# Half of the hidden product moved between the score products of a solu/MoE kernel

## What is computed

```python
# attention: B, H, S, D = 4, 8, 768, 48
for t in range(S):
    S_re, S_im = ar * S_re - ai * S_im + kv[t], ar * S_im + ai * S_re
    y[t] = q[t] @ S_re
# dense layer: 3072 tokens, d_model 384, d_ff 1024
h = x @ w_in
e = exp(h - max(h));  solu = h * e / sum(e)
ln = (solu - mean) / sqrt(var + 1e-6) * g_ln
x = ln @ w_out
# experts: 8, hidden 1024, each token goes to its best two
out[token] += weight * (relu(x @ w1[e]) @ w2[e])
```

## Time and profile before

| | |
|---|---|
| median of 3 runs | 1293.69 us (1292.68 to 1297.07) |
| profiled execution, whole time | 1297.07 us |
| its span | 1295.3 us |
| TensorE busy | 1098.5 us (85%) |
| VectorE busy | 871.4 us (67%) |
| ScalarE busy | 621.1 us (48%) |
| mean granted TensorE clock | 0.942 of full |

### The profile page before, as it was taken

How to read it: one execution, slowest core, us unless ns; L and a number is a source line. 1 busy time by engine, 2 the same in 40 slices (tenths; PEclk the granted TensorE clock), 3 DMA queues, 4 the chain that set the end, 5 groups by cost and what they waited for, 6 DMA issues and landing times.

```text
span 1295.3 us, 21866 instructions
## 1 busy us (share of the span) xinstructions
PE 1098.5 (85%) x7864; PEld 982.9 (76%) x7864; DVE 871.4 (67%) x1715; ACT 621.1 (48%) x964; POOL 446.2 (34%) x416
## 2 busy tenths in 40 slices
PE   0016889988988988999995299999999999999996
PEld 0015667766766767777884299999999999999996
DVE  4849649948957966974542467777767776767772
ACT  4331454455445455353432255555555555555551
POOL 3020131224234233423342424444344444444431
PEclk9976979989989998999997599999999999999998
DMA  9320031130112021011110667677767776766740
GB/s 254 122 73 19 19 92 40 36 92 26 50 41 77 25 62 32 26 48 46 50 20 13 221 203 250 230 232 248 244 225 250 251 230 239 237 228 221 242 159 1
DMA packets 85979, 167.50 MB, mean 129 GB/s; under 512 B 18566, under 2 KB 57696, under 8 KB 85872
## 3 DMA queue, kind: packets, MB, share of 16 engines
q1 hardware_dynamic: 72432, 137.71, 33.5%
q0 software_dynamic: 13440, 28.40, 6.2%
HBM read 148.83 MB, written 21.92 MB: 132 GB/s over the span
## 4 chain that ended last, share of the span: by engine, by line
PE 52%; DVE 3%; issue 1%; ACT 1%; DMA 1%; POOL 1%; SPq 0%; POOLq 0%; DVEq 0%; ACTq 0%
PE bank L1301 21%; PE bank L1482 20%; PE bank L1358 3%; PE bank L1327 3%; PE bank L1292 2%; PE bank L1349 1%; PE bank L1397 1%; PE bank L1399 1%; PE bank L1426 0%; DVE turn L941 0%; DMA mine<-tags 0%; POOL tags L568 0%; DMA xg<-xs,mine 0%; DVE zl L1104 0%; PE bank L1379 0%
## 5 line engine op out<-in xcount | busy, mean ns | idle before, releaser
L854 ACT ACTIVATE hh<-bank 128x256 fp32r<-128x256 f32 x248 | 95.3, 384 | 253.9 <-PE bank L1301 253.9
L1301 PE MATMUL bank<-sxh,w1h 128*128 128x256 f32 x744 | 212.2, 285 | 1.9 <-DVE sxl L1247 1.9
L1301 PE MATMUL bank<-sxh,w1l 128*128 128x256 f32 x744 | 210.5, 283 | 0.0
L1301 PE MATMUL bank<-sxl,w1h 128*128 128x256 f32 x744 | 210.2, 282 | 0.0
L1270 DVE SCALAR_TENSOR_TENSOR hl<-bank,hh 128x256 fp32r<-128x256 f32 x248 | 104.8, 423 | 117.4 <-ACT hh L854 117.4
L646 POOL DMA_INDIRECT out<-yo,mine x62 | 77.9, 1257 | 275.9 <-DVE yo L1263 266.5
L1482 PE MATMUL bank<-w2h,hh 128*128 128x384 f32 x496 | 167.5, 338 | 0.0
L1482 PE MATMUL bank<-w2l,hh 128*128 128x384 f32 x496 | 166.7, 336 | 0.0
L1482 PE MATMUL bank<-w2h,hl 128*128 128x384 f32 x496 | 166.5, 336 | 0.0
L1301 PEld LDWEIGHTS bank<-sxh,w1h 128*128 128x128 f32 x744 | 140.6, 189 | 2.3 <-DVE sxl L1247 2.3
L1301 PEld LDWEIGHTS bank<-sxh,w1l 128*128 128x128 f32 x744 | 141.7, 190 | 0.0
(11 more groups left out here) (183 smaller groups left out, 2427.2 us busy)
## 6 DMA issues: line engine op xcount, KB each, us to landing
raw<-in_w SPq DMA_DIRECT2D x62, 1536.0 KB, 7.0
ar<-in_a_re SPq DMA_DIRECT2D x6, 768.0 KB, 4.5
turn<-in_a_im SPq DMA_DIRECT2D x6, 768.0 KB, 5.8
qk<-in_q SPq DMA_DIRECT2D x48, 96.0 KB, 2.4
qk<-in_k SPq DMA_DIRECT2D x48, 96.0 KB, 2.5
out<-wide SPq DMA_DIRECT2D x9, 512.0 KB, 11.4
vt<-in_v SPq DMA_DIRECT2D x24, 192.0 KB, 2.7
xs<-x SPq DMA_DIRECT2D x24, 192.0 KB, 2.7
```

Source lines behind the costliest of these rows:

```text
L854: nc.scalar.activation(hh[:, f % NH, :], bank[:, f % 2, 0:CAP], ACT.Relu).then_inc(hh_done, 1)
L1301: ins = MM(dst, stationary[a_](cc), moving[b_](cc), start=(n_ == 0), stop=(n_ == len(terms) - 1))
```

## The change

The hidden products are issued in two parts. The first half (12 products, bank 4) stays in front of the waits for the scores. The second half (12 products, bank 5) goes behind those waits, in three groups of four between the four pairs of score products; where there is no tile m, all of it follows directly. The group after p_ = 2 holds the last hidden product, which raises h_mm, so h_mm comes before the last quarter of the scores. a_mm is raised by the last score, as before.

```diff
-                    hidden(0, 6 * NP)
+                    hidden(0, 3 * NP)
                 if has(m):
 
                     pe.wait_ge(qp_done, 2 * (m + 1))
@@
-                    ins.then_inc(a_mm, 1)
+                        if p_ == NP - 1:
+                            ins.then_inc(a_mm, 1)
+                        else:
+                            hidden(3 * NP + NP * p_, 3 * NP + NP * (p_ + 1))
+                else:
+                    hidden(3 * NP, 6 * NP)
```

## The result

The changed kernel takes 1364.81 us (median of 4 runs, 1352.96 to 1370.98) against 1293.18 us beside it: 71.6 us slower by these medians. The ratio 1.0512 (95% interval 1.0428 to 1.0599), some 66 us, is that of the fast runs: it leaves out one execution in the slower state, 1370.98 us, and takes in three more, the profiled one among them. The forecast was slower, 1330 us, with a range of 1312 to 1348. The direction holds; the size is about twice the forecast. The profiled execution took 1354.94 us (span 1353.2), one of the quicker ones.

A forecast was written before the change was run, and what follows sets the result against it. TensorE's program order was taken to set the pace of most first-phase tiles, VectorE's queue in some. Terms 13.8 + 9.4 + 16.2 - 4 = +35.4 us, 36 added to the median 1293.69: about 1330 us, range 1312 to 1348.

The forecast's parts named there:

- The wait for zl moves: TensorE waits behind 12 hidden products instead of 24; where zl is late, 2.76 us more idle: 13.8 + 9.4 us.
- bodies of the first kind: Bodies 4, 8, 12, 16, 20, where zl is late; delay paid in full, 5 x 2.76 = 13.8 us.
- the second kind: Bodies 5, 9, 13, 17, zl late by less; some 0.4 us of slack before xl, so 9.4 us.
- Passages: Three added round trips a tile between hidden products and scores, 0.3 us each: 18 x 0.9 = 16.2 us.
- the last bodies: Bodies 21 to 24, nothing prepared for a later chunk, no wait for zl; expected to grow about 0.9 us each.
- The rival of free passages: Switching between scores and hidden products costs nothing: 1313 us, chance 0.12.
- h_mm later: The nmax reduction on VectorE starts later, covered by ScalarE's at; costed at nothing.
- TensorE's clock: Low clock after late zl stays as before; body 4's long low stretch becomes less likely: credit of 4 us.
- the clock turns against it: Longer pauses keep TensorE low through scores, half the hidden products and into the result part: 1353 us, chance 0.10.
- Absorbed: VectorE and ScalarE take up the delay in bodies 5, 9, 13, 17: 1320 us, chance 0.08.
- faster: Scores run under neighbouring hidden products in 18 tiles: 1284 us, chance 0.04.
- no change: Same overlap at about 1.2 us a tile, or gain and loss of like size; chance 0.04.

The follow-up runs named there:

- the single trip alone: Changed kernel with the second half of the hidden products as one block between score pairs 0,1 and 2,3: 1327.68 us, +37.9 against the kernel before.
- scores in one block: Kernel before with 12 hidden products ahead of the waits, then all scores unbroken, then the other 12 hidden products: 1326.84 us, +37.0.
- The two partial kernels: The new order only in the nine bodies where zl is late (1340.54 us, +49.5), or only in the other bodies (1315.27 us, +24.3).
- wait only: Kernel before with the waits moved behind 12 hidden products, the other 12 next, then the scores unbroken: 1317.33 us, +27.5.
- thin groups: Kernel before with 21 hidden products ahead of the waits and a single one in each of three gaps between score pairs: 1375.74 us, +85.9.
- the state block: State products issued together ahead of the result products: kernel before 1283.38 us, with zl early 1274.44, thin groups 1323.21, changed kernel 1338.11.

## Why the prediction was wrong in size

- **The wait for zl moves.** Right in place and size of the wait: 54.4 us in nine times, forecast 54. The price was forecast at 13.8 + 9.4 = 23.2 us; moved alone it costs 27.5. In that kernel the bodies of the first kind (but for body 4, whose long low stretch did not come) grew from xl to xl by some 3.5 instead of 2.76 us and the second kind by 2.9 to 3.7 instead of 2.4, because the 12 hidden products behind the pause run at 1.2 GHz: 5.05 us in body 12 instead of 2.76, 2.3 us lost, where the scores lost 1.7 before.
- **Passages.** 0.3 us a trip, measured 0.37 in the last bodies; 0.9 us a tile against 1.15. The bounds of 0.2 and 0.41 a trip hold there; the single trip alone cost 0.52, above them. That bodies 6, 10, 14 and 18 are covered by VectorE's queue was wrong: they pay 0.95 us through the slower pieces beside GpSimd. 18 x 1.15 + 4 x 0.95 = 24.5 us instead of 16.2. The rule of the Trainium skill ("TensorEngine Tiling (Array Packing)", Key Properties: a change of tiling mode drains TensorE) agrees with this: the 0.37 us stand in the trace, and the order that adds no change between 64 and 112 rows (scores in one block) left the period at 17.68 us. The rival of free passages has fallen.
- **h_mm later.** The wait before nmax is there in 20 bodies, and in the last bodies it costs nothing, as said: they grow by the trips alone.
- **TensorE's clock. This is the step that failed.** The prediction read from body 9 that the low stretch ends some 3.4 us after work resumes, left it at that for the new order, expected long stretches to become less likely because a block twice as long stands behind the wait, and credited 4 us. In the alternated block the clock stayed low for 4.1 to 10.2 us. In the two profiles that costs 29.8 - 12.4 = 17.4 us, near the 15 us that the prediction gave as the other end (low for twice as long); the absence of body 4's long stretch gives 5 of it back, for which the prediction had reckoned 6.7. So a loss of 12.4 us stands where a gain of 4 was entered. On the medians, 71.6 - 27.5 - 24.5 = 19.6 us is left for the clock (14 by the ratio), worked out and not measured by itself. The two partial kernels place it: in the nine late bodies 49.5 - 27.5 - 9 x 1.15 = 11.7 us, in the others 24.3 - 9 x 1.15 - 4 x 0.95 = 10.1 (differences of medians, so good to a few us). The rival "the clock turns against it" had 0.10 and 1353 and came nearest. Its size was about right; its cause was not, since it put the low clock down to the longer pauses, and these alone left it low for no more than 5.1 us.
- **Absorbed, faster, no change:** fell. Nothing was absorbed in bodies 5, 9, 13 and 17, which grew by 4.6 to 6.4 us from xl to xl.
- **Direction.** It is right by the terms that were right: the wait alone costs 27.5 us.

What is shown: the pause alone does not make the loss (wait only), and behind the thin groups it was the order in which state and result products were issued that decided whether the clock came back in the result part (thin groups with and without the block). It is not so in every body: in body 5 of the kernel before the clock came back at 209.49 us, some 2 us into the alternated result part (0.50 granted over 207.60 to 209.45, 1.00 over 209.55 to 212.00), in body 4 only after it. What in an alternated stretch keeps the clock low stays open, and so do the 10 us outside the late bodies. And the length of a low stretch varies from run to run: the changed kernel's runs lie 18 us apart.

## What to carry to other kernels

Before splitting a block of matmuls around a wait, ask what cover the block gave that wait: cover taken away is paid in full wherever the wait was already late, and here a pause of 2.4 us was already followed by the low clock. Behind a pause, compare an unbroken block with an alternated one: here the same products in two blocks had the clock back after 4.1 to 5.1 us, and in seven pieces after 4.1 to 10.2. At full clock alternating still cost 0.3 to 0.5 us a trip. Here the order was not the thing to mend: making zl earlier on VectorE gave 16.6 us, and it is the fastest kernel of this study at 1274.41 us, together with the one that adds the state block (1274.44).

## Not expected of the hardware

- Changing between 112-row and 64-row products cost 0.37 us a round trip at full clock (three trips; a single one 0.52), and between 48-column and full-width products 0.34, in work that has no wait in it. Changing between 112-row and 128-row products cost nothing that shows.
- After a pause of 5.7 us TensorE stayed at 1.2 GHz for 20.4 us of work without a break, while two kinds of product were issued in turn; with the same pause and one of the two alternations taken out, it was 9.3 us.
- Four VectorE pieces of 384 columns took 1.96 us alone, 3.31 and 4.84 us when two or three of GpSimd's tensor operations lay beside them; the nmax reduction of the same body, which reads PSUM, took 1.22 us both with GpSimd's mask beside it (before) and without (after).
